# Moving a turn of the token rows across the loop edge, and a split in between the squares, on the vector engine of a mixture-of-experts kernel

## The reference

```
# 1 attention: k and v averaged over groups of 8 keys, 4 batches, 8 heads, 576 tokens, 64 wide
scores = scale * q @ k_pooled.T ; attn = softmax(scores) ; x = attn @ v_pooled      -> x is 2304 x 512
# 2 experts: for each token the two best of 8 experts by noisy gate logits
out[mask] += top2_w[mask, k] * (relu(x[mask] @ w1[e]) @ w2[e])   # w1[e] 512x1024, w2[e] 1024x512
# 3 dense: h = x @ w_in (2048 wide); g = max(0.01*h, h); out = g @ w_out
```

## Time and profile before

| | us |
|---|---|
| median of 3 runs | 1028.03 |
| the profiled execution's own time | 1028.59 |
| its span from first to last instruction | 1026.9 |
| PE busy | 983.4 (96%) |
| DVE busy | 679.1 (66%) |
| ACT busy | 246.9 (24%) |
| POOL busy | 398.9 (39%) |

### The profile page before, as it was taken

One profiled execution on the slowest core, in us unless ns is written; L12 is line 12 of the kernel. 1 busy time (PEld: TensorE's weight loads), 2 busy tenths in 40 slices (PEclk: granted clock), 3 DMA queues, 4 the chain that ended last, 5 costly groups with the idle time before them and its releaser, 6 DMA issues.

```text
span 1026.9 us, 16478 instructions
## 1 busy us (share of the span) xinstructions
PE 983.4 (96%) x4710; PEld 824.4 (80%) x4711; DVE 679.1 (66%) x1325; ACT 246.9 (24%) x455; POOL 398.9 (39%) x453
## 2 busy tenths in 40 slices
PE   5998778999999999999999999999999999999998
PEld 4988656788888888888888877888888888888886
DVE  5877658999999999999999975433333324333222
ACT  3543111221211211211212113322222223222222
POOL 6488881190928374654637059301000100000000
PEclk9988789999999999999999999999999999999999
DMA  8945552162535344342525135211011101001001
GB/s 299 336 179 206 193 183 86 42 187 78 157 109 143 109 135 123 120 145 93 169 84 165 61 103 154 63 41 41 21 46 37 33 9 62 21 1 41 0 1 41
DMA packets 72792, 105.82 MB, mean 103 GB/s; under 512 B 9520, under 2 KB 32176, under 8 KB 72752
## 3 DMA queue, kind: packets, MB, share of 16 engines
q1 hardware_dynamic: 35456, 63.59, 19.9%
q10 hardware_dynamic: 31536, 22.82, 7.1%
q0 software_dynamic: 5760, 18.88, 5.6%
HBM read 77.21 MB, written 28.05 MB: 103 GB/s over the span
## 4 chain that ended last, share of the span: by engine, by line
PE 45%; DVE 34%; issue 11%; ACT 5%; POOL 2%; DMA 2%; ACTq 1%; DVEq 0%; SPq 0%; POOLq 0%
DVE ps L1326 24%; PE ps L734 13%; PE ps L735 13%; PE ps L736 13%; DVE hT_lo L1344 3%; DVE xs_lo L1313 3%; PE ps L687 2%; ACT hT_hi L1001 2%; ACT y_sb L1017 2%; PE ps L663 2%; POOL w_split L553 1%; PE ps L673 1%; DMA xs<-x_sorted 1%; PE ps L838 1%; POOL w_split L551 1%
## 5 line engine op out<-in xcount | busy, mean ns | idle before, releaser
L1326 DVE STREAM_TRANSPOSE ps<-ps 32x256 f32<-32x256 f32 x672 | 313.0, 466 | 14.1
L553 POOL TENSOR_TENSOR w_split<-w_raw,w_split 128x512 fp32r<-128x512 f32 x144 | 186.5, 1295 | 12.0
L1534 DVE TENSOR_TENSOR g_sb<-h_small,ps 128x512 f32<-128x512 f32 (+1 forms) x80 | 50.8, 634 | 192.8 <-ACT h_small L1118 191.1
L551 POOL TENSOR_SCALAR w_split<-w_raw 128x512 fp32r<-128x512 f32 x144 | 91.2, 634 | 181.8 <-PE ps L736 181.4
L734 PE MATMUL ps<-w_split,xs_hi 128*128 (+1 forms) x344 | 137.2, 399 | 14.1 <-DVE xs_lo L1313 13.3
L734 PE MATMUL ps<-w_split,hT_hi 128*128 (+1 forms) x344 | 134.2, 390 | 3.2 <-DVE hT_lo L1344 3.2
L736 PE MATMUL ps<-w_split,xs_lo 128*128 (+1 forms) x344 | 136.6, 397 | 0.0
L735 PE MATMUL ps<-w_split,xs_hi 128*128 (+1 forms) x344 | 136.3, 396 | 0.0
L736 PE MATMUL ps<-w_split,hT_lo 128*128 (+1 forms) x344 | 133.9, 389 | 0.0
L735 PE MATMUL ps<-w_split,hT_hi 128*128 (+1 forms) x344 | 133.8, 389 | 0.0
L610 POOL DMA_INDIRECT y_in<-y_blocks,y_rows x36 | 35.0, 971 | 246.5 <-DVE x L1487 200.8
(11 more groups left out here) (176 smaller groups left out, 1362.6 us busy)
## 6 DMA issues: line engine op xcount, KB each, us to landing
w_raw<-in_wall_dram SPq DMA_DIRECT2D x160, 256.0 KB
xs<-x_sorted ACTq DMA_DIRECT2D x176, 64.0 KB
y_blocks<-y_sb ACTq DMA_DIRECT2D x43, 256.0 KB, 2.2
k_raw<-in_kT_dram SPq DMA_DIRECT2D x16, 288.0 KB, 5.3
q_sb<-in_qT_dram SPq DMA_DIRECT2D x18, 256.0 KB, 5.1
v_raw<-in_vT_dram SPq DMA_DIRECT2D x16, 288.0 KB, 5.9
out_dram<-h_sb SPq DMA_DIRECT2D x10, 256.0 KB, 2.0
x_sorted<-zero_rows SPq DMA_DIRECT2D x9, 256.0 KB, 4.2
```

Of the source, the lines that this page charges most:

```text
L551: pool.tensor_scalar(hi, w_raw[:, a, :], 1.0, 0.0, ALU.mult, ALU.add).then_inc(split_hi, 1)
L553: pool.tensor_tensor(lo, w_raw[:, a, :], hi.bitcast(F32), ALU.subtract).then_inc(split, 1)
L1326: ins = dve.transpose(ps[a * QUAD:(a + 1) * QUAD, HT_BANK:HT_BANK + 2, :] .rearrange("p n (k t i) -> p (n k) t i", t=QUADS, i=QUAD)[:, :, ...
L1534: dve.tensor_tensor(g_sb[:, f % 2, 0:n], h_small[:, f % 2, 0:n], ps[:, H2_BANK + f % 2, 0:n], ALU.max).then_inc(g_made, 1)
```

## The change

In the DVE program `turn_rows` moves from before `split_half(b, 0)` at the end of an iteration to the head of the next one, behind `split_half(b, 0)`, and its block number falls by one with it (`b + 2` there is `b + 1` here). `split_rows(b + 1)` moves from between `turn_front` and `turn_back` to behind the first two squares of `turn_back`. A turn of a block that does not exist, number 43, is no longer made, and the wait of PE for it goes.

```
             with pe.Fori(LISTED_BY, BLOCKS) as b:
                 up(b, expert_of(b))
                 down(b - 1, expert_of(b - 1), False)
-            pe.wait_ge(xs_turned, BLOCKS + 1)
             down(BLOCKS - 1, EXPERTS - 1, False, True)
...
-            def turn_back(b):
+            def turn_back(b, rows):
                 dve.wait_ge(h_summed, b * 2 + 2)
-                turn_squares([(a, t) for a in (2, 3) for t in range(QUADS)]).then_inc(h_turned, 1)
+                turn_squares([(2, 0), (2, 1)])
+                if rows:
+                    split_rows(b + 1)
+                turn_squares([(2, 2), (2, 3), (3, 0), (3, 1), (3, 2), (3, 3)]).then_inc(h_turned, 1)
...
             turn_front(1)
-            split_rows(2)
-            turn_back(1)
+            turn_back(1, True)
             split_half(1, 0)
             split_half(1, 1)
             turn_front(2)
-            turn_back(2)
+            turn_back(2, False)
             split_half(2, 0)
             turn_rows(3)
             split_rows(3)
-            turn_rows(4)
             for b in range(3, LISTED_BY):
+                turn_rows(b + 1)
                 split_half(b - 1, 1)
...
                 turn_front(b)
-                split_rows(b + 1)
-                turn_back(b)
-                turn_rows(b + 2)
+                turn_back(b, True)
                 split_half(b, 0)
             with dve.Fori(LISTED_BY, BLOCKS - 1) as b:
+                turn_rows(b + 1)
                 split_half(b - 1, 1)
                 turn_front(b)
-                split_rows(b + 1)
-                turn_back(b)
-                turn_rows(b + 2)
+                turn_back(b, True)
                 split_half(b, 0)
```

More of the change, by code:

```diff
@@ L1492, in _ @@
             turn_front(BLOCKS - 1)
-            turn_back(BLOCKS - 1)
+            turn_back(BLOCKS - 1, False)
             split_half(BLOCKS - 1, 0)
```

## The result

The changed kernel takes 1042.76 us (median of 4 runs, 1039.69 to 1045.74), the kernel before 1028.31 in the same rounds: a ratio of 1.0136 (95% interval 1.0108 to 1.0163). The forecast was 1043.0, from 1037.5 to 1048.5. The profiled execution took 1042.48, its span is 1040.8, 13.9 longer than before. Further runs of the changed kernel stand on record: all 13 lie between 1038.72 and 1045.74.

What follows compares the result with a forecast made beforehand. DVE's own chain was taken to bound the blocks. 14.1 us for the loop plus 0.7 for PE's clock made 14.8 on 1028.59, 1043.4 for the profiled execution; the median forecast was 1043 us, range 1037.5 to 1048.5.

Steps and rivals of the forecast that it cites:

- The cover: Loop: the 0.73 us turn was almost free under the relu wait; moved, DVE idles 0.67 us before the front half's split.
- The distances: DVE loop: back half's split 0.63 us after the turn, not 0.75; next squares at T + 2.84, period up 0.38 us.
- Count: Loop: 38 turns stand behind a front half's split, block 5 loses nothing, so 37 times 0.38 = 14.1 us.
- The loop's branch and the transfers: Loop: exposed branch between 0 and 5.9 us, taken as 0; no wait for row transfers, 0.
- Rival A: Loop: a longer turn, distance 0.75, costs 18.5 us, 1047.2; with all of the branch 1053; chance 17%.
- B: Loop: instruction pairs overlap better, period grows only 0.26 us, 9.6 us in all, 1037.6 or 1038.3; chance 11%.
- C: Loop: PE sets the period and DVE only follows, time stays 1028; chance 5% together with smaller ways to a gain.
- D: Loop: PE's two short waits each period bring half clock, some 35 us more, 1078; chance 3%.
- E: Loop: the later split of the rows frees DVE of a wait for `xs_hi`; gain put at 0, sum unchanged.
- PE's waits: Loop: PE waits about 0.35 us a block, on the turned squares and on `xs_lo`.
- Ahead of the loop: Block 2's `up` would start 0.96 us later, waiting for the split of the rows; between 0 and 0.96, taken as 0.
- The last down: Before the last `down`, PE idle grows from 2.23 to 3.1 us; half clock behind it costs 0 or 1.3, taken as 0.7.

Runs made afterwards that it cites:

- turn_only: The kernel before with only the turn of the rows moved, the split of the rows left between eighth and ninth square: 1048.01 us, ratio 1.0191.
- the two fillings: The changed kernel with one extra vector addition per loop pass: before the front half's split (1043.62 us), or between back half's split and front squares (1067.55 us).
- relu_first_before: The kernel before with ACT's copy of y in the loop moved from between the two relus to behind them: 1027.41 us, ratio 0.9992.
- squares_reversed: The kernel before with the back half's squares of each row of squares in reversed order: 1026.83 us, one run.
- split_only: The kernel before with only the split of the rows moved behind the tenth square, the turn left in place: 1028.28 us, ratio 1.0004.
- filled_elsewhere: The changed kernel with an extra 128x512 vector addition per loop pass between the back half's split and the front squares: 1067.55 us.
- filled_gap: The changed kernel with the same extra vector addition per loop pass in the gap between last square and front half's split: 1043.62 us.

## Why the prediction was right

*What bounds the kernel.* Right: DVE's own chain decided the end of the blocks, and what was added arrived whole. Shown by turn_only and the two fillings, and by 37 x 0.356 = 13.2 us of period against 13.13 of loop. But it is the bound by little: without its wait for the second relu DVE's chain takes 10.60 us a block and PE's 10.88 decides (relu_first_before).

*The cover.* Right: 0.67 us of idle before the front half's split, none before the back half's. The idle time predicted from two places outside the loop is the one found inside to 0.01.

*The distances.* Predicted T + 2.84 for the squares and 0.38 a period; measured T + 2.83 at this place and 0.356 on average. The choice of 0.63 over 0.75 was right, but not for the first reason given for it, that the relu was long over there and late in the other pair: in squares_reversed the relu ends as late as before, and the distance is 0.63. The second reason holds. The Trainium skill's rule ("VectorE: DVE Perf Modes", section "Two Vector instructions with no wait between them") had it so, and the trace agrees: 0.63 us where the last PSUM input read began in the same group of partitions, 0.75 where in another. The page puts it a little more strictly than I did: every input of the instruction counts, and an output is compared with the last output into the same memory. In these rows both come to the same.

*Count.* 37 periods: right. Block by block the front half's split falls back by 0.35 to 0.36 us from block 3 to 4 and in each of the 36 steps from 5 to 41, which makes 37, and by nothing from 4 to 5, as forecast. The loop's branch and the transfers: 0, right. Rival A falls by the distance, B and C by the period, D because PE's short waits came 35 times and the period holds no lost clock. E's gain was none, as split_only shows.

*PE's waits.* Half wrong. I had PE waiting twice a block, on `xs_lo` and on the squares. It waits for `xs_lo` alone, 0.18 us and a slow first matmul; that starts the second half of `up` late enough for the squares to be there. In turn_only the wait stands at the second half instead, and the time of the loop is the same: where PE waits follows from DVE's order, how long from DVE's period.

*Ahead of the loop.* I took 0 out of 0 to 0.96. The squares of block 2 waited 0.23 us for PE:

```profile
153.34 6.69 DVE L1325 STREAM_TRANSPOSE ps<-ps 32x256 f32<-32x256 f32 x14 [0.23 <-PE ps L736]
```

The turn of block 4 comes 0.10 us later in this trace. That can't be put down to the change: from the first turn of rows to this one three traces of the changed kernel take 50.01, 50.09 and 50.78 us, the trace before 49.67.

*The last down.* The term that was mis-sized. I took half of 1.3 us, as if it might or might not happen. It happened in all eight traces, at 1.3 to 2.8 us; and in the profiled run part 3 gave back 0.65 us, which I had not in the sum. Idle time grew by 0.6, not by 0.9 us.

The sum was 14.8 for the profiled execution, and 13.9 were found: 1.0 too much in the loop, 0.6 too little in the last down, 0.65 of return left out, 0.1 ahead of the loop. These misses partly cancel. That the median came within 0.3 us of the 1043 is luck, since runs of the kernel differ by 7; the mechanism and the loop's 13.13 us for 14.1 are not.

## What to carry to other kernels

When an engine must wait for the answer of another, look at what stands between question and answer: an independent instruction there is free up to the length of the wait, and moved elsewhere it costs, in each pass, its length less whatever other waits it then covers (here 0.36 of 0.73 us). Two engines with nearly equal periods (10.86 and 10.88) leave little slack for that; which of them decides is seen at the end of the loop, where the faster one still makes the other wait. And where runs scatter by several us, compare stretches of the traces and not medians: here the loop's repeats to 0.1 us in a kernel whose runs differ by 7.

## What was not expected of the hardware

A vector addition and GpSimd's work stretch each other. The extra instruction of filled_elsewhere takes 0.67 or 0.68 us in 16 of its 37 passes, and in each of these GpSimd is idle; it takes 1.10 to 1.30 in the other 21, and in each of these GpSimd splits weights beside it. GpSimd, ahead of and beside the one at 264.26 (start, us, instruction, idle before):

```profile
259.04 0.62 POOL L551 TENSOR_SCALAR w_split<-w_raw 128x512 fp32r<-128x512 f32 x1 [27.00 <-PE ps L736]
...
263.67 1.29 POOL L553 TENSOR_TENSOR w_split<-w_raw,w_split 128x512 fp32r<-128x512 f32 x1
264.93 1.06 POOL L551 TENSOR_SCALAR w_split<-w_raw 128x512 fp32r<-128x512 f32 x1
```

It had been idle for 27 us up to 259.04, and so during the one at 252.69, which took 0.67; and its own instruction at 264.93 takes 1.06 where its like takes 0.62, so both lose.

In filled_gap 21 of the 37 stand beside GpSimd's work too, but only seven are stretched (0.95 to 0.97). In the other 14 the addition takes 0.67 and it is GpSimd's instruction that is long, about 2.0 us instead of 1.29 or 1.3 to 1.5 instead of 0.62. So either of the two can be the one that loses (GpSimd's durations in a profile are rough). The kernel's turns and splits do not show it: in the rows above a turn takes 0.73 and a split of h 0.67 to 0.69. They read at most one operand from SBUF, the extra instruction two. By the Trainium skill ("VectorE: DVE Perf Modes", section "Two Vector instructions with no wait between them") the second SBUF input comes through a read interface that is shared with GpSimd, and the traces fit that. Moving GpSimd's work away from the addition wasn't tried, so the cause is read from these times and not tested.

The spread. Runs of the changed kernel went from 1038.72 to 1045.74, and the kernel before from 1024.47 to 1038.88 in the 23 runs of one session. In the traces of one kernel the loop differs by 0.1 us; the granted clock of PE from 55 to 125 us was 0.80 in the trace before, 0.76 and 0.72 in the two above, and the start of the first block lies between 111.67 (filled_elsewhere) and 122.71 us (turn_only). And the length of a stretch at half clock behind one and the same idle time: of the eight last downs five took 14.6 to 14.9 us, three 16.0 to 16.1.
